# Turning, sorting and table layout rewritten in an attention and two-mixture kernel

## What is computed

```
# x (8,8,512,64), state (8,8,32,64); scale = 1/8
xread = softmax(scale * x @ state^T) @ state
sread = softmax(scale * state @ x^T) @ x
x = concat([xread, sread], rows), heads side by side      # 4352 tokens x 512
# first mixture, soft: phi (512,32), 8 experts with 4 slots each
logits = x @ phi
slot_in = softmax(logits, over tokens)^T @ x
slot_out[e] = relu(slot_in[e] @ w1[e]) @ w2[e]            # w1 512x1024, w2 1024x512
x = softmax(logits, over slots) @ slot_out
# second mixture, hard: one expert a token
e = argmax(x @ w_gate)
out = max_prob * sigmoid(x @ w_output_gate)[e] * (relu(x @ v1[e]) @ v2[e])
```

## Time and profile before

| | us |
|---|---|
| median of 3 runs | 518.16 (517.82 to 519.98) |
| the profiled execution | 520.96 |
| its span, first to last instruction | 519.2 |
| PE busy | 454.6 (88%) |
| mean granted clock of TensorE | 0.941 of full |

### The profile page before, as it was taken

How to read it: one execution, slowest core, us unless ns; L and a number is a source line. 1 busy time by engine, 2 the same in 40 slices (tenths; PEclk the granted TensorE clock), 3 DMA queues, 4 the chain that set the end, 5 groups by cost and what they waited for, 6 DMA issues and landing times.

```text
span 519.2 us, 9941 instructions
## 1 busy us (share of the span) xinstructions
PE 454.6 (88%) x3705; PEld 241.8 (47%) x3706; DVE 132.7 (26%) x315; ACT 127.7 (25%) x329; POOL 127.8 (25%) x191
## 2 busy tenths in 40 slices
PE   7888786799898793999999999999999999999991
PEld 5676655663435462444444444444444444444440
DVE  2689698820004601101010101010101010101000
ACT  3978554300001101212121212121212121212110
POOL 2433513040021004032222222232323232323110
PEclk9999898789796966999999999999999999999997
DMA  8799546779999998678601010101010101010110
GB/s 284 251 348 296 212 164 203 286 281 391 432 425 428 427 394 283 232 231 294 232 22 43 22 43 22 43 22 43 22 43 21 43 22 42 26 39 24 38 44 3
DMA packets 29306, 87.20 MB, mean 168 GB/s; under 512 B 5942, under 2 KB 15704, under 8 KB 26200
## 3 DMA queue, kind: packets, MB, share of 16 engines
q1 hardware_dynamic: 24016, 76.65, 39.3%
q0 software_dynamic: 3952, 9.49, 5.4%
q10 hardware_dynamic: 1304, 0.57, 0.4%
HBM read 77.25 MB, written 9.75 MB: 168 GB/s over the span
## 4 chain that ended last, share of the span: by engine, by line
PE 66%; DMA 14%; ACT 5%; issue 5%; DVE 5%; SPq 2%; POOL 1%; ACTq 0%; POOLq 0%; DVEq 0%
PE bank L858 48%; DMA token_rows<-z 5%; DMA arena<-in_moe_w 5%; DMA arena<-in_x 3%; PE bank L846 3%; PE bank L741 2%; SPq L287 2%; ACT z L1015 2%; PE bank L529 1%; PE bank L835 1%; DMA z<-token_rows,sidx 1%; PE bank L789 1%; PE bank L518 1%; PE bank L570 1%; PE bank L592 1%
## 5 line engine op out<-in xcount | busy, mean ns | idle before, releaser
L858 PE MATMUL bank<-arena,z 128*128 x560 | 249.3, 598 | 15.6 <-ACT z L1015 10.1
L858 PEld LDWEIGHTS bank<-arena,z 128*128 128x128 f32 x560 | 103.6, 190 | 139.6 <-issue 139.6
L1313 DVE TENSOR_SCALAR z<-bank 128x256 f32<-128x256 f32 x70 | 26.4, 419 | 260.2 <-PE bank L846 260.2
L1022 ACT ACTIVATE z<-bank,tile_gate 128x512 f32<-128x512 f32 x35 | 24.0, 687 | 242.0 <-PE bank L858 242.0
L449 POOL COPY rows_to<-sidx 128x1 int32 (+1 forms) x35 | 6.3, 181 | 167.9 <-ACT z L1022 167.9
L468 POOL DMA_INDIRECT out<-z,rows_to x35 | 36.7, 1049 | 29.8 <-POOL rows_to L449 29.8
L453 POOL DMA_INDIRECT z<-token_rows,rows_from x32 | 33.6, 1050 | 25.6 <-POOL rows_from L449 25.6
L846 PE MATMUL bank<-cT,parts 32*128 32x128 f32 x560 | 26.0, 300 | 0.0
L1015 ACT ACTIVATE z<-bank 128x256 f32<-128x256 f32 x70 | 23.0, 381 | 3.1 <-PE bank L846 1.1
L835 PE MATMUL bank<-ident,z 128*32 128x128 f32 x280 | 15.4, 292 | 9.1 <-DMA z<-token_rows,sidx 9.1
L846 PEld LDWEIGHTS bank<-cT,parts 32*128 32x128 f32 x560 | 19.2, 189 | 7.7 <-issue 7.7
(11 more groups left out here) (205 smaller groups left out, 416.5 us busy)
## 6 DMA issues: line engine op xcount, KB each, us to landing
arena<-in_moe_w SPq DMA_DIRECT2D x29, 2048.0 KB, 12.1
arena<-in_x SPq DMA_DIRECT2D x7, 1024.0 KB, 8.8
parts<-in_moe_w SPq DMA_DIRECT2D x3, 2048.0 KB, 13.1
arena<-in_x SPq DMA_DIRECT2D x2, 512.0 KB, 5.7
out<-z,rows_to POOLq DMA_INDIRECT x35, 3.0
token_rows<-z ACTq DMA_DIRECT2D x1, 528.0 KB
z<-in_state SPq DMA_DIRECT2D x1, 512.0 KB, 3.6
z<-in_state SPq DMA_DIRECT2D x8, 64.0 KB, 8.2
```

Of the source, the lines that this page charges most:

```text
L858: mm = e.matmul(pY[p][:, :], hT[p][:, c, :], arena[:, bass.ds(ex * UNIT + 512 * c, 512)], start=(c == 0), stop=(c == CF - 1))
L1022: e.activation(ysb[p], pY[p][:, :], ACT.Copy, scale=tile_gate[:, q:q + 1])\
L1313: e.tensor_scalar(hT[p][:, 2 * g:2 * g + 2, :], bank[g][:, 0:GW].rearrange("p (c t) -> p c t", c=2), 0.0, None, ALU.max).then_inc(relu_v, 1)
```

## The change

- **Loop, PE.** A step now starts with the expert load and the waits for the relus, the free bank and v2 (`output_free`); then come the turning of tile t+2, hidden of t+1, and the output, with no wait between the last two. The waits of hidden for the relus are gone, since those ahead cover them. `turn_c` is one 128x128 transpose, its source `c4` being the 32 weights laid out four times by DVE (`turned_rows`), which waits for the gathered row in PE's place.
- **Loop, others.** The two relus of a tile raise their semaphore once. The row to scatter to is no longer read from `sidx` but is a 34th number of each table row, which ACT copies with the gate (`gate_to`); ACT's slot is free when POOL has copied the row number rather than when the result is copied.
- **Table.** Rows lie in the order of the partitions, so ACT writes one run of 34 x 34 numbers a partition in one DMA. The first 102 rows are a stand-in for places without a token (gate 0, row out of bounds), written by SP early on.
- **Sorting.** Per token column, DVE makes `lane_hot` and `tile_row` (place times a coded row number) in two operations, 68 in all, in place of three large ones; the weights of the sort matmul are now unit-stride and 41 columns wide instead of 82; PE takes each column as it comes. POOL's wide copy of the lanes is gone.
- **Order.** The expert count stands after the first v1 product instead of the second.
- **Foldings.** ACT and DVE write `siP`, `hP`, `soP` chunk by chunk, so that L720, L749 and L764 read unit-stride weights.
- **Fillers.** Three groups of transposes of the identity (4, 4, 6) are added around the last folding and the gate logits.
- **Loads.** Each of the first four weight loads is cut into four DMAs of 4 KB a partition.

```diff
-                if ex == 1:
+                if ex == 0:
                     count_experts()
...
             def turn_c(t, q, wait=True):
                 if wait:
                     e.wait_ge(c_copied, t)
-                e.wait_ge(row_in[q], 4 * (t - q) + 16)
-                for g in range(4):
-                    mm = e.matmul(pC[NS * g:NS * g + NS, :], row[q][:, 0:NS], ident[:, :], start=True, stop=True)
-                mm.then_inc(c_psum, 1)
+                e.wait_ge(c4_ready, t + 1)
+                e.transpose(pC, c4[q % 2], ident[:, :]).then_inc(c_psum, 1)
...
-            def output(t, p, wait=True):
-                ex = expert(t)
-                e.wait_ge(v2_ready, ex + 1)
-                e.wait_ge(relu_a, 2 * t + 2)
-                e.wait_ge(relu_v, 2 * t + 2)
+            def output_free(t, ex, wait=True):
+                e.wait_ge(relu_a, t + 1)
+                e.wait_ge(relu_v, t + 1)
                 if wait:
                     e.wait_ge(y_copied, t - 1)
+                e.wait_ge(v2_ready, ex + 1)
+
+            def output(ex, p):
...
             def step(t, q, first=False):
+                ex = expert(t)
+                output_free(t, ex, wait=not (first and q < 2))
...
-                output(t, q % 2, wait=not (first and q < 2))
+                output(ex, q % 2)
...
             def sort_rows():
 
-                e.wait_ge(lane_ready, 3)
                 for t in range(NT):
-                    mm = e.matmul(pT[:, 0:2 * ST], lane_hot[:, :, t], tile_id[:, :, :, t], start=(t == 0),
-                                  stop=(t == NT - 1))
+                    e.wait_ge(lane_ready, 2 * t + 2)
+                    mm = e.matmul(pT[:, 0:ST], lane_hot[:, t, :], tile_row[:, t, :], start=(t == 0), stop=(t == NT - 1))
...
+            for t in range(NT):
+                e.tensor_scalar(lane_hot[:, t, :], lane[:, :], dlane[:, t:t + 1], None, ALU.is_equal)\
+                 .then_inc(lane_ready, 1)
+                e.tensor_scalar(tile_row[:, t, :], lane[:, 0:ST], dtile[:, t:t + 1], code_f[:, t:t + 1], ALU.is_equal,
+                                ALU.mult).then_inc(lane_ready, 1)
...
+            def turned_rows(t, q):
+
+                e.wait_ge(row_in[q], 4 * (t - q) + 16)
+                if not isinstance(t, int) or t >= 2:
+                    e.wait_ge(c_psum, t - 1)
+                e.tensor_copy(c4[q % 2].rearrange("p (g n) -> p g n", g=4),
+                              row[q][:, 0:NS].unsqueeze(1).to_broadcast([P, 4, NS])).then_inc(c4_ready, 1)
...
-            e.wait_ge(row_ready, 2)
-            by_batch = table.rearrange("(b r) w -> b r w", b=NB)
-            for f in range(2):
-                e.dma_start(by_batch[4 * f:4 * f + 4, S:S + NS, :], rowbuf[:, NB * J + f, :]).then_inc(table_out, 16)
-            e.dma_start(by_batch[:, 0:S, :].rearrange("b (p j) w -> p b (j w)", j=J),
-                        rowbuf[:, 0:NB * J, :].rearrange("p (b j) w -> p b (j w)", b=NB)).then_inc(table_out, 16)
+            e.wait_ge(row_ready, 3)
+            e.dma_start(table[FIRST_ROW:TABLE, :].rearrange("(p t) w -> p (t w)", p=P), z2[:, 0:NT * ROWW]).then_inc(table_out, 16)
...
-                mm = e.matmul(pF[:, NS * c:NS * c + NS], every(siP, c, CD), foldn[:, :], start=True, stop=True)
+                mm = e.matmul(pF[:, NS * c:NS * c + NS], siP[:, P * c:P * c + P], foldn[:, :], start=True, stop=True)
...
+                rows = src[ex].rearrange("(p c) n -> p (c n)", p=P)
+                step = UNIT // pieces(u)
+                for a in range(0, UNIT, step):
+                    e.dma_start(slot(SLOT[u])[:, a:a + step], rows[:, a:a + step]).then_inc(w_in[SLOT[u]], 16)
```

More of the change, by code:

```diff
@@ L41 @@
 GW = F // 4
-ROWW = NS + 1
+ROWW = NS + 2
 GATE_W = NS
+LEAD = 3
+FIRST_ROW = LEAD * NT
+TABLE = FIRST_ROW + NT * P
+EARLY = 4
 NOROW = 1 << 20
@@ L102, in build @@
         hTm = z1[:, 0:2080]
[L103 to L105 removed]
+        lane_hot = z1[:, 0:NT * P // 2].bitcast(BF16).rearrange("p (t l) -> p t l", t=NT)
+        tile_row = z1[:, NT * P // 2:NT * P // 2 + NT * ST // 2].bitcast(BF16).rearrange("p (t s) -> p t s", t=NT)
+        c4 = [z1[:, 2880 + P * q:2880 + P * q + P] for q in range(2)]
         z2 = sb("z2", [P, 2560])
@@ L237, in build, with pieces @@
                   + [(v1, e, CD) for e in range(NE)])
+        def pieces(u):
+            return 4 if u < EARLY else 1
         def w_loaded(u):
-            return 16 * sum(1 for v in range(u + 1) if SLOT[v] == SLOT[u])
+            return 16 * sum(pieces(v) for v in range(u + 1) if SLOT[v] == SLOT[u])
         def live_tile(e, live, t):
@@ L432, in _ @@
             e.tensor_copy(rowbuf[:, :, 0:NS], comb).then_inc(row_ready, 1)
+            e.tensor_copy(rowbuf[:, :, GATE_W + 1], rowid[:, :]).then_inc(row_ready, 1)
             e.wait_ge(sit_psum, 1)
             e.memset(hTm, 0.0).then_inc(ht_zero, 1)
[L437 to L450 removed]
+            e.wait_ge(sidx_ready, 1)
+            e.wait_ge(table_out, 16 * 2)
+            last_row, last_out = e.to_reg(TABLE - 1), e.to_reg(ROWS - 1)
             def gather_row(q, rows):
@@ L457, in gather @@
                 e.wait_ge(gate_saved, t - 3)
-                numbers(rows_from[:, q:q + 1], t, from_copied, t - 3)
+                e.sem_inc(turns, 1)
+                src = sidx[:, t:t + 1] if isinstance(t, int) else sidx[:, bass.ds(t, 1)]
+                e.tensor_copy(rows_from[:, q:q + 1], src).then_inc(from_copied, 1)
+                e.wait_ge(from_copied, t - 3)
                 e.sem_inc(gathers, 1)
@@ L748, in _ @@
             for c in range(CF):
-                mm = e.matmul(pE[:, NS * c:NS * c + NS], every(hP, c, CF), fold[:, 0, :], start=True, stop=True)
+                mm = e.matmul(pE[:, NS * c:NS * c + NS], hP[:, P * c:P * c + P], fold[:, 0, :], start=True, stop=True)
             mm.then_inc(ht_psum, 1)
@@ L761, in _ @@
                 mm.then_inc(w_used, 1)
+            keep_clock(4)
             e.wait_ge(so_copied, 1)
             for c in range(CD):
-                mm = e.matmul(pT[:, P * c:P * c + P], every(soP, c, CD), fold[:, :, :], start=True, stop=True)
+                mm = e.matmul(pT[:, P * c:P * c + P], soP[:, P * c:P * c + P], fold[:, :, :], start=True, stop=True)
             mm.then_inc(sot_psum, 1)
+            keep_clock(4)
             e.wait_ge(sot_ready, 1)
@@ L772, in _ @@
             mm.then_inc(g2_psum, 1)
+            keep_clock(6)
             e.wait_ge(g2_ready, 4)
@@ L868, in step @@
                         hidden(t + 1, (q + 1) % 2)
-                output(t, q % 2, wait=not (first and q < 2))
+                output(ex, q % 2)
             turn_c(0, 0, wait=False)
             turn_c(1, 1)
-            hidden(0, 0, wait=False)
+            hidden(0, 0)
             keep_clock(10, pL)
```

129 lines of the change are left out of this document (54 added, 75 removed).

## The result

| | before | changed |
|---|---|---|
| median of 4 runs, us | 518.2 (517.82 to 519.98) | 488.89 (485.99 to 490.71) |
| the profiled execution, us | 520.96 | 490.71 |
| its span, us | 519.2 | 488.9 |
| PE busy, us | 454.6 | 430.6 |
| mean granted clock | 0.941 | 0.967 |

The ratio is 0.9423, 95% interval 0.9368 to 0.9478. 487.5 was forecast, with 482 to 498 as the range; the profiled execution took 490.71 where the working had 490.3.

The account below looks back on a forecast made before the run. PE bounds the loop and the landing of v2[1] the start: 23.0 + 7.6 = 30.6 us off the profiled 520.96 gives 490.3, less 2.8 for the median 487.5 us, range 482 to 498.

Parts of the forecast that it names:

- The gap goes: Loop, PE between hidden and output: load and waits moved ahead of the turning cost nothing, 0.47 us a step gone.
- The turning: Loop: one transpose of 0.12 us replaces eight column-tile passes of 0.35 us, saving 0.23 us a step.
- The step: Loop, output to output: 7.06 + 0.12 + 0.70 = 7.88 us instead of 8.61, over 31 steps 22.6 us.
- v2[1] bounds the start: Before the first output: expert 1's v2 load, holding the first tile's expert, lands at 201.1; output 1 begins 7.6 us sooner.
- D: Early part: cut loads bring a later x 2 to 5 us sooner, 483 to 485, chance 0.12; or delay it, 490 to 492, 0.06.
- Half clock: First output: after PE idles some 4 us the clock is at half, adding 1.0 to 1.2 us to output 0.
- All else is there by then: Start: routing, sort (`sidx` by 188), last v1 product, table and gathers (by 199) are all ready before v2[1].
- A: Loop: the gap is the array's and stays; only the turning's 7.3 us go, 14.9 in all, 503; chance 0.08.
- B: Loop: the sequencer's lead is too short, the turning comes late by up to 0.47 us; 495 at half; chance 0.14.
- C: Loop: gathered rows land over 10 us after issue and block DVE; 630 us at 15 us to land; chance 0.02.
- E: Whole kernel: nothing gained, the start held by something not seen and the gap kept; chance 0.01.

Follow-up runs that it names:

- waits_alone: The kernel before with only the expert load and the output's waits moved ahead of the turning, hidden's own relu waits gone: 500.92 us, ratio 0.9636.
- turning_in_four: The changed kernel with the one transpose replaced by four products with the identity, 32 columns each: 495.58 us, ratio 0.9550.
- uncut_loads: The changed kernel with the first four weight loads whole again: 484.99 us, ratio 0.9345.
- folds_strided: The changed kernel with siP, hP and soP laid as before and the foldings reading strided weights: 490.99 us, ratio 0.9413.

## Why the prediction was right, and where two errors met

**The gap goes: right.** The step named the load and the waits and took its evidence from the tail. 0.0 us of idle time remain, and `waits_alone` shows it without any other part. Forecast for the gap and the overlap together were 0.50 us a step (1.20 to 0.70); it was 0.54.

**The turning: right in sum.** 0.12 us for the transpose was to save 0.23; 0.23 came in the rows, and taking it back in `turning_in_four` cost 0.25. In the rows the turning begins 6.97 us after the output, not 7.06, and takes 0.21: the split was off, the sum was not.

**The step: 7.83 for 7.88.** Over 31 steps the loop gave 24.2 us where 22.6 was forecast, and the last step 0.43 for 0.37. The term was mis-sized by the 0.05 us of overlap between hidden and output.

**v2[1] bounds the start: right. Its time: wrong by 2.2 us.** The step said 201.1, from 202.07 less 1.0 for the folding, less 0.5 for the table, plus 0.5 for the gathers, cut loads nothing. In the profiled execution it was 203.3. Of the 2.2 us, 1.6 lie ahead of the w2 issue (108.34 against 106.70) and 0.6 behind it. Behind it the folding is the term that failed: it was put ahead of the queue of loads because it stands ahead of the slot releases, but the queue starts at the w2 issue, before it, and the whole stretch shrank by some 0.4 us in place of 1.0. The 0.5 us for the table and the 0.5 against it for the gathers were not tested one by one. Ahead of it, the cut loads were given nothing, with a chance of 0.12 for sooner and 0.06 for later; later by 2 us is what `uncut_loads` shows by the medians, so D had the right place and the wrong favourite. The rest is scatter: the w2 issue at 108.34 in that execution, 104.06 and 104.68 in two others, which had v2[1] near 199 and took 486.19 and 486.89 us instead of 490.71. A single execution of each kernel, compared as the working did, can miss by that much in this term.

**Half clock: right.** Output 0 was to begin 1.6 us after v2[1] and output 1 9.1 after that, 10.7 in all; it was 1.1 and 9.3, 10.4. Windows of the changed kernel (columns as above):

```profile
200.00:204.00 4.00, 0.66 (x13) 0.54 (x17) 0.00 (x0) 0.29 (x2) 0.00 (x0) 1.00 0.49 179
204.00:208.00 4.00, 4.00 (x17) 1.88 (x14) 1.17 (x4) 0.73 (x3) 0.00 (x0) 0.57 0.84 241
208.00:212.00 4.00, 4.00 (x10) 1.71 (x9) 0.00 (x0) 0.00 (x0) 0.00 (x0) 1.00 0.75 284
```

PE idles from 198.9 to 203.3, and the clock shows half only in the window that follows, 0.57; turning and hidden were still near full speed (0.33 and 0.88 us, where 0.24 and 1.24 were forecast). That is why output 0 came 0.5 us earlier behind v2[1] than said; the output lost 1.5 us to the clock (8.63 for 7.13) where 1.0 to 1.2 was said.

**All else is there by then: right.** `sidx` at 185.49 (at most 188 was said, near 185 looked for), the last v1 product's end at 194.1 (193.7), the table before the first gather.

**The sum.** 30.6 was forecast for the profiled execution and 30.25 measured: 1.6 us too little from the loop, 1.9 too much from the start. The closeness is partly luck; each part alone missed by that much.

**The rivals.** A, the array's gap, fell: by the rule cited from the Trainium skill ("TensorE: Matmul & The Clock Gate", Part 3, The mechanism) weights of all rows would have had to wait for hidden's quarter of the rows. `waits_alone` has 0.0 us of idle time ahead of the 477 matmuls of some 30 outputs, each of which begins behind a hidden, so the trace does not bear the rule out here; the same section also lets a weight load go ahead into a background weight buffer, which the rival left out. The row of the first hidden had said so, and so does the output itself: its matmuls and their weights all use every row, and each next weight load of 0.19 us lies within the 7.13 us in which PE is never idle. B, the lead too short, fell: nothing is idle ahead of L848 in the loop, though load, register work and all the waits stand there now. C, late rows, fell: rows were late for DVE in two steps, by 2.9 us together, and none of it passed on to PE. E fell with the result.

## What to carry to other kernels

A register load or a wait costs nothing while its engine still has long work in flight, and is exposed behind short work (0.34 to 0.47 us here); look for a place where the same instructions show no gap, and move them there. When a load is late, find the first issue from which the queue has no hole: only what stands ahead of that issue moves the load, and shortening work inside the stretch buys next to nothing. Cut a load only if someone uses its first piece; each piece is an issue more on the queue's engine, and the loads behind it came later.

## What the runs showed of the hardware

- The length of the last wait did not set what the clock's fall cost. In `uncut_loads` PE was idle for 2.88 us, the granted clock was at half from about 196 to 202.5 us, and turning, hidden and much of the output (9.50 us) ran at it; in the changed kernel it was idle for 4.46 us, the clock was at half only from 204 to 207, turning and hidden ran nearly at full and the output took 8.63. `folds_strided` (2.89 us idle) had 9.41, `turning_in_four` (2.50) 8.07. Why is open.
- Filler transposes of the identity held the granted clock at full over 5.46 us in which PE had nothing else to do, and the output behind them ran in 7.13 us.
- DMA engines at nearly the same busy share (1.06 and 1.10) moved 304 and 345 GB/s from 10 to 20 us, with cut loads and without.
- Eight foldings of 128x128 weights took 1.05 us with unit-stride weights and 2.02 to 2.05 us with weights 4 elements apart.
- The stretch from the w2 issue to v2[1], some 95 us of nearly full DMA engines, repeated within 0.4 us in nine of eleven profiles with the new table, while the 100 us ahead of it scattered by over 4 for one and the same kernel.
